# An attention layer and two feed-forward layers on one core: more steps with two banks, statistics in halves, weight tiles in other steps, a packed mask, and a third value part formed by VectorE

## The reference

```python
s_g = scale * q_g @ k_all.T;  out_g = softmax(s_g) @ v_all          # k_all = [k_g, k_l]
s_ll = where(|i - j| <= 32, scale * q_l @ k_l.T, -1e9)
out_l = softmax([scale * q_l @ k_g.T, s_ll]) @ [v_g, v_l]
x = concat([out_g, out_l], axis=2)   # heads side by side: (4, 544, 512)
x = x + relu(layernorm(x) * g @ w_ch1) @ w_ch2                      # 512 -> 2048 -> 512
h = relu(x @ w_in)                                                  # 512 -> 1024
out = (h * sigmoid(conv3_along_sequence(h, conv_w))) @ w_out
```

## Time and profile before

| | us |
|---|---|
| median of three runs | 797.08 (796.56 to 798.47) |
| the profiled execution, its own time | 794.28 |
| its span, first to last instruction | 792.5 |
| TensorE busy | 747.4 (94% of the span) |
| VectorE busy | 414.7 (52%) |
| ScalarE busy | 341.0 (43%) |
| GpSimd busy | 286.1 (36%) |
| mean granted TensorE clock | 0.98 of full speed |

### The profile page before, as it was taken

How to read it: one execution, slowest core, us unless ns; L and a number is a source line. 1 busy time by engine, 2 the same in 40 slices (tenths; PEclk the granted TensorE clock), 3 DMA queues, 4 the chain that set the end, 5 groups by cost and what they waited for, 6 DMA issues and landing times.

```text
span 792.5 us, 16702 instructions
## 1 busy us (share of the span) xinstructions
PE 747.4 (94%) x6496; PEld 690.6 (87%) x6496; DVE 414.7 (52%) x1008; ACT 341.0 (43%) x854; POOL 286.1 (36%) x241
## 2 busy tenths in 40 slices
PE   3886799989999999999999999999999999999997
PEld 2785789988998999899998999888888999999997
DVE  4798765685557654542112131212237676676764
ACT  5897576656565654143212222111114434343343
POOL 4888766353445340043212343020102222222322
PEclk9996799999999999999999999999999999999999
DMA  8766765355534600336261684650524222220200
GB/s 231 201 183 186 229 174 170 94 184 149 148 89 140 203 26 27 96 114 194 66 199 54 164 234 134 160 189 27 160 84 117 76 86 77 67 83 32 86 30 28
DMA packets 92702, 98.84 MB, mean 125 GB/s; under 512 B 10832, under 2 KB 68304, under 8 KB 92624
## 3 DMA queue, kind: packets, MB, share of 16 engines
q1 hardware_dynamic: 92624, 97.78, 41.5%
HBM read 68.14 MB, written 29.62 MB: 123 GB/s over the span
## 4 chain that ended last, share of the span: by engine, by line
PE 82%; DVE 7%; ACT 4%; issue 3%; POOL 2%; DMA 1%; SPq 0%; ACTq 0%; POOLq 0%; DVEq 0%
PE u_ps L506 34%; PE y_ps L506 23%; PE s_ps L506 15%; PE t_ps L548 5%; PE o_ps L506 4%; DVE bst L800 1%; DVE m_sb L731 1%; DVE p_lo L746 1%; DVE ln_n L815 1%; POOL k_lo L1095 1%; DVE v_res L722 1%; POOL q_st L1102 1%; ACT p_hi L969 1%; ACT e_sb L943 1%; DMA k_raw<-in_kqT 1%
## 5 line engine op out<-in xcount | busy, mean ns | idle before, releaser
L837 DVE SCALAR_TENSOR_TENSOR hb<-u_ps,hb 128x384 fp32r<-128x384 f32 (+1 forms) x48 | 28.9, 602 | 176.2 <-ACT hb L1013 176.2
L1131 POOL TENSOR_TENSOR hb<-gated,hb 128x272 fp32r<-128x272 f32 x64 | 54.9, 859 | 154.0 <-ACT hb L1041 154.0
L1013 ACT ACTIVATE hb<-u_ps 128x384 fp32r<-128x384 f32 (+1 forms) x48 | 25.3, 527 | 176.1 <-PE u_ps L506 176.1
L506 PE MATMUL u_ps<-xc,w_hi 128*128 128x274 f32 x512 | 99.8, 289 | 0.0
L854 DVE SCALAR_TENSOR_TENSOR conv_h<-relu_h,conv_sb,conv_h 128x272 f32<-128x272 f32 x128 | 88.8, 694 | 4.5
L1095 POOL TENSOR_TENSOR k_lo<-k_raw,k_hi 128x736 fp32r<-128x736 f32 x31 | 58.7, 1894 | 79.1 <-ACT k_hi L925 77.8
L506 PE MATMUL u_ps<-xn,w_hi 128*128 128x256 f32 x448 | 86.5, 291 | 0.1
L1116 POOL TENSOR_TENSOR w_lo<-w_raw,w_hi 128x1024 fp32r<-128x1024 f32 x24 | 57.8, 2409 | 79.1 <-ACT w_hi L1003 79.1
L506 PEld LDWEIGHTS u_ps<-xc,w_hi 128*128 128x128 f32 x512 | 80.8, 189 | 0.2
L1027 ACT ACTIVATE relu_h<-u_ps 128x274 f32<-128x274 f32 x64 | 25.6, 400 | 120.7 <-PE u_ps L506 120.7
L506 PE MATMUL u_ps<-xc,w_lo 128*128 128x274 f32 x256 | 73.9, 289 | 0.0
(11 more groups left out here) (135 smaller groups left out, 2148.7 us busy)
## 6 DMA issues: line engine op xcount, KB each, us to landing
w_raw<-in_wall SPq DMA_DIRECT2D x24, 512.0 KB, 4.0
k_raw<-in_kqT SPq DMA_DIRECT2D x64, 184.0 KB, 3.4
xc<-y_parts SPq DMA_DIRECT2D x8, 1092.0 KB, 5.9
q_raw<-in_kqT SPq DMA_DIRECT2D x64, 136.0 KB, 2.9
v_raw<-in_vx SPq DMA_DIRECT2D x32, 260.0 KB, 3.4
y_parts<-yT SPq DMA_DIRECT2D x16, 512.0 KB, 3.7
xn_parts<-xn SPq DMA_DIRECT2D x14, 512.0 KB, 4.1
xb<-xn_parts SPq DMA_DIRECT2D x14, 512.0 KB, 6.6
```

The source lines that it names most:

```text
L506: return nc.tensor.matmul(out, lhsT, rhs, start=start, stop=stop)
L837: v.scalar_tensor_tensor(out=lo, in0=u_ps[n % 2][:, 0:width], scalar=0.0, in1=hi.bitcast(f32), op0=ALU.max, op1=ALU.subtract).then_inc(hlo ...
L1131: g.tensor_tensor(hb[sc % HSLOTS][:, 1, 0:CN], gated[sc % 2][:, :], hb[sc % HSLOTS][:, 0, 0:CN].bitcast(f32), ALU.subtract).then_inc(clo_o ...
```

## The change

- **Banks.** The second transpose bank is used for all transposes of steps below 23 (before: below 19), the second output bank up to output number 10 (before: 8).
- **Statistics.** `ln_sums` is split: `half_sums` takes the sums of 256 of the 512 columns after the first four heads (steps 11, 27, 43, 59) and of the other 256 in steps 19, 35, 51, 67; `variances` combines both.
- **Weight tiles.** The first eight are treated in steps 9, 12, 15, 17, 24, 25, 26 and 28, through three staging buffers; the third is the memory of `y1_sb`.
- **Mask.** It comes from the host as bf16 in three tiles and is loaded straight into place by one transfer of 192 KB in place of two of 256 KB and two casts.
- **Value parts.** `v_last` moves from GpSimd to VectorE, in the same odd steps, ahead of `half_sums` and `scale_up`. GpSimd's `q_low` no longer waits for it.
- **Transfers.** The first four query transfers are issued by ScalarE. The last output is stored in four transfers, each as its part is copied.

```diff
-T_BANK = [k % 2 if T_STEP[k] < 19 else 0 for k in range(len(T_SEQ))]
+T_BANK = [k % 2 if T_STEP[k] < U0 else 0 for k in range(len(T_SEQ))]
...
-O_FLIP = 8
+O_FLIP = 10
...
-W_STEP = [13 + 2 * j for j in range(8)] + [70 + 2 * j for j in range(8)] + [U0 + N1 + 4 + 2 * j for j in range(8)]
+W_STEP = ([9, 12, 15, 17, 24, 25, 26, 28] + [70 + 2 * j for j in range(8)]
+          + [U0 + N1 + 4 + 2 * j for j in range(8)])
+W_SLOT = [j % 3 for j in range(8)] + [j % 2 for j in range(16)]
...
-        maskb = sb(ctx, "maskb", [P, 2, 512], bf16)
+        maskb = sb(ctx, "maskb", [P, 3, 256], bf16)
-        bst = sb(ctx, "bst", [P, QT, 6])
+        bst = sb(ctx, "bst", [P, QT, 2, 6])
...
             def w_load_step(j):
-                return 7 if j < 2 else W_STEP[j - 2] + 2
+                return 3 + 2 * j if j < 3 else W_STEP[W_BEFORE[j]] + 2
...
+                else:
+                    for m in range(KT):
+                        sp.wait_ge(oe_ok, KT * cc + m + 1)
+                        sp.dma_start(outT[b][:, m, CN * c:CN * (c + 1)], y_sb[:, m, :]).then_inc(out_out, 16)
...
-            load_q(0)
             load_k(0)
-            for u in range(2):
-                sp.dma_start(mask_raw[u], maskp[:, u, :]).then_inc(mask_in, 16)
+            sp.dma_start(maskb[:, :, :].bitcast(f32), maskp).then_inc(mask_in, 16)
             load_k(1)
-            load_q(1)
...
+            def v_last(m):
+                r = m % VSLOTS
+                dve.wait_ge(vres_ok, m + 1)
+                v.tensor_tensor(low(v_res[r]), v_res[r][:, :], top(v_res[r]), ALU.subtract).then_inc(vend_ok, 1)
...
+            def half_sums(b, half):
+                dve.wait_ge(o_ok, o_head(HEADS * b + GH * half + 3) + 1)
+                if half == 0 and b > 0:
+                    dve.wait_ge(lnn_ok, QT * b)
+                for t in range(QT):
+                    v.bn_stats(bst[:, t, half, :], x_loc[b % 2][:, t, 256 * half:256 * (half + 1)]).then_inc(stat_ok, 1)
...
+                if s % 2 == 1 and s // 2 < NHEADS:
+                    v_last(s // 2)
                 if s % 2 == 0 and 0 <= (s - 4) // 2 < NHEADS:
                     read_out((s - 4) // 2)
+                if s % 16 == 11 and s // 16 < BATCH:
+                    half_sums(s // 16, 0)
                 if s % 16 == 3 and 1 <= s // 16 <= BATCH:
-                    ln_sums(s // 16 - 1)
+                    half_sums(s // 16 - 1, 1)
+                    variances(s // 16 - 1)
...
+            for m in range(2):
+                act.dma_start(q_raw[m][0:D, :], kqT[m, :, KW:KQW]).then_inc(q_in[m], 16)
+                act.dma_start(q_raw[m][D:P, :], kqT[m, :, KW:KQW]).then_inc(q_in[m], 16)
...
-                if s % 2 == 1 and s // 2 < NHEADS:
-                    v_last(s // 2)
-                    if (s + 4) // 2 < NHEADS:
-                        pool.wait_ge(vend_ok, s // 2 + 1)
-                        q_low((s + 4) // 2)
+                if s % 2 == 1 and (s + 4) // 2 < NHEADS:
+                    pool.wait_ge(klo_ok, (s + 3) // 2)
+                    if min(W_STEP) < s:
+                        pool.wait_ge(wlo_ok, sum(step < s for step in W_STEP))
+                    if s % 16 == 3 and 1 <= s // 16 <= BATCH:
+                        pool.wait_ge(rstd_ok, s // 16)
+                    q_low((s + 4) // 2)
```

More of the change, by code:

```diff
@@ L143, in stats_before @@
 def stats_before(b):
-    return 9 * b
-W_STEP = [13 + 2 * j for j in range(8)] + [70 + 2 * j for j in range(8)] + [U0 + N1 + 4 + 2 * j for j in range(8)]
+    return 13 * b
+W_STEP = ([9, 12, 15, 17, 24, 25, 26, 28] + [70 + 2 * j for j in range(8)]
+          + [U0 + N1 + 4 + 2 * j for j in range(8)])
 W_AT = {s: j for j, s in enumerate(W_STEP)}
+W_SLOT = [j % 3 for j in range(8)] + [j % 2 for j in range(16)]
+W_USE = [W_SLOT[:j + 1].count(W_SLOT[j]) for j in range(24)]
+W_BEFORE = [max([i for i in range(j) if W_SLOT[i] == W_SLOT[j]], default=-1) for j in range(24)]
 def attention_mlp(nc, kqT, vx, wall, gln, convw, ident, maskp, outT):
@@ L194, in attention_mlp @@
         h_lo = [sb(xs, f"h_lo{r}", [P, 2 * P], f32r) for r in range(HSLOTS)]
-        y1_sb = [sb(xs, f"y1_sb{r}", [P, DM]) for r in range(2)]
+        y1_sb = sb(xs, "y1_sb", [P, 2, DM])
+        w_raw.append(y1_sb[:, :, :].rearrange("p a b -> p (a b)"))
         x_glo = sb(xs, "x_glo", [P, D])
@@ L249, in attention_mlp @@
         yb = [y_ps[:, 0, :], y_ps[:, 1, :], s_ps[:, 0, :], s_ps[:, 1, :]]
-        mask_raw = [v_res[VSLOTS - 2 + u][:, 0:512] for u in range(2)]
         def g_ps(G):
             return y_ps if G < 2 else s_ps
-        mask_in, const_in, const_ok, mask_ok = sem("mask_in"), sem("const_in"), sem("const_ok"), sem("mask_ok")
+        mask_in, const_in, const_ok = sem("mask_in"), sem("const_in"), sem("const_ok")
         warm_ok = sem("warm_ok")
@@ L260, in attention_mlp @@
         v_in = [sem(f"v_in{r}") for r in range(VSLOTS)]
-        w_in = [sem(f"w_in{r}") for r in range(2)]
+        w_in = [sem(f"w_in{r}") for r in range(3)]
         khi_ok, qhi_ok, qghi_ok = sem("khi_ok"), sem("qhi_ok"), sem("qghi_ok")
@@ L998, in weights_hi @@
                     act.wait_ge(dn_ok, DN[N1])
-                raw = w_raw[j % 2]
+                raw = w_raw[W_SLOT[j]]
                 if j < 2 * HALF:
@@ L1106, in q_low @@
                 g.tensor_tensor(to, q_raw[m % 2][D:P, SL:S], to.bitcast(f32), ALU.subtract).then_inc(qglo_ok, 1)
-            def v_last(m):
-                r = m % VSLOTS
-                pool.wait_ge(vres_ok, m + 1)
-                g.tensor_tensor(low(v_res[r]), v_res[r][:, :], top(v_res[r]), ALU.subtract).then_inc(vend_ok, 1)
             def weights_lo(j):
@@ L1115, in weights_lo @@
                 pool.wait_ge(whi_ok, j + 1)
-                g.tensor_tensor(w_lo[at][:, :], w_raw[j % 2][:, :], w_hi[at][:, :].bitcast(f32),
+                g.tensor_tensor(w_lo[at][:, :], w_raw[W_SLOT[j]][:, :], w_hi[at][:, :].bitcast(f32),
                                 ALU.subtract).then_inc(wlo_ok, 1)
@@ L1120, in inverse_deviation @@
                 n = 1 if b == BATCH else QT
-                pool.wait_ge(stat_ok, stats_before(b) + 2 * n + 1)
+                pool.wait_ge(stat_ok, stats_before(b) + (3 if b == BATCH else 13))
                 g.tensor_tensor(rstd[:, 0:n], veps[:, 0:n], minus_half[:, 0:n], ALU.pow).then_inc(rstd_ok, 1)
```

68 lines of the change are left out of this document (32 added, 36 removed).

## The result

The changed kernel takes 802.34 us (median of 4 runs, 801.4 to 803.67), the kernel before beside it on the same chip 796.82 us (796.51 to 798.47). The ratio is 1.0071, with a 95% interval of 1.0054 to 1.0088: slower, where 791.6 us was forecast. The profiled execution has a span of 799.5 us, 7.0 more than before.

What follows compares the result with a forecast made beforehand. TensorE, busy 94% of the span, was taken as the bound, with the time to `up(0)` to be won. Terms -1.4 + 1.0 - 5.0 - 1.0 + 1.9 - 1.0 = -5.5 from 794.28, plus 2.8, gave 791.6 us; range 786 to 799.

Steps and rivals of the forecast that it cites:

- Value part, steps 3 to 16: Steps 3 to 16: GpSimd relieved of `v_last`, VectorE's added work just fits; +1.0 us, from -2 to +5.
- "slower" rival: Steps 3 to 22: VectorE becomes the bound as `v_last` waits for GpSimd subtractions; +8, in all 799.6 us; chance 0.15.
- Opening: Before step 3: keys arrive earlier with fewer transfers ahead; -1.4 us, between 0.5 (bytes decide) and 2.5 (issue decides).
- Steps 17 to 22: Banks, halved statistics and moved weight tiles shorten the chain before `up(0)`; -5.0 us, from -2 to -8.
- Step 25: G0's transposes no longer wait 1.12 us for a low part behind a weight cast; -1.0 us.
- Step 30: `up(7)` waits for weight tile 7, only two steps after its `scale_up`; +1.9 us, bounds +0.5 and +3.
- Steps 35, 51, 67: Halved statistics -1.1, `v_last` ahead +0.6: -0.5 us each in steps 35 and 51, nothing in 67.
- End: Last output stored in four transfers: issues start earlier, last lands about the same; 0, within 0.5 us either way.
- The clock rival: Steps 17 to 22: fewer waits give TensorE its full 2.4 GHz; 3.5 us more gain, 788 us; chance 0.20.

Runs made afterwards that it cites:

- e1: Changed kernel with `v_last` back on GpSimd in the same steps, all else as changed: 796.39 us, 0.9985 of the kernel before.
- e5: Changed kernel with `v_last` back on GpSimd and the first eight weight tiles in steps 13, 15, ... 27 as before: 790.18 us, 0.9919 of the kernel before.
- e11: Changed kernel with `v_last` on GpSimd and weight tiles in steps 9, 11, 15, 17, 24 to 27: 789.21 us, 0.991 of the kernel before.
- e9: Kernel before with `v_last` replaced by a one-input `bn_stats` on VectorE, third value part left out: 800.01 us, 1.0037 of the kernel before.
- e10: Changed kernel with `v_last` replaced by a one-input `bn_stats` on VectorE, third value part left out: 797.55 us, 1.0017 of the kernel before.
- e6: Kernel before with the bank changes alone (transpose banks and output bank flips): 795.07 us, 0.9984 of the kernel before.
- e4: Changed kernel with the first eight weight tiles in their old steps 13, 15, ... 27, three staging buffers kept: 798.7 us, 1.002 of the kernel before.
- e3: Changed kernel with weight tile 7 treated in step 27 in place of 28: 798.79 us, 1.0022 of the kernel before.
- e2: Kernel before with `v_last` moved to VectorE alone: 805.96 us, 1.0109 of the kernel before.
- e7: Changed kernel with `v_last` on VectorE in the even steps, right behind `v_residue`: 834.7 us, 1.0481 of the kernel before.
- e12: Changed kernel with `v_last` on GpSimd and weight tiles in steps 13, 15, 17, 19, 24 to 27: 789.27 us, 0.9909 of the kernel before.
- e8: e5 with a 416-byte pad that puts later buffers at their addresses in the kernel before: 788.51 us, 0.9905 of the kernel before.

## Why the prediction was wrong

**The step that failed** is the term "*Value part, steps 3 to 16*", +1.0 with bounds of -2 and +5. It measured +10.0, outside its bounds and 9.0 of the 12.5 us between the forecast sum (-5.5) and the measured span (+7.0). Three things were off in it.

- *The wait of `v_last`.* I let it meet "the last 0.3 to 0.5 us" of a subtraction. The mean over ten was 0.54 us, but it is made of six that lose 0.3 or less, one that loses 0.6 and three that lose 1.3: each meeting costs what is left of the other's instruction. I had the row that shows this, 2.15 us for a `scale_up`, and spread it thin.
- *The waits of the others.* I charged the wait to `v_last` alone. In steps 3 to 16 its seven lose 3.8 us, but the three `scale_up` lose 3.7, two of them because they stand right behind a `v_last` and GpSimd's waiting operation goes in between. 6.3 us of added work, and 3.8, 3.5 more than before, and 0.3 of `v_residue` make 13.9; VectorE's busy time rose by 13.3.
- *The weight tiles.* I costed the one tile more as 1.05 us of ScalarE and one `scale_up`. e1 against e5 says 7.6 us in steps 3 to 16 without any `v_last` on VectorE. e11 splits it: 4.0 are tile 1's even step, 3.6 are left for the added tile and the earlier places.

My "slower" rival had the right mechanism with a mean wait of 0.9 us and 799.6 us; the mean was 0.54, so by its own arithmetic it would not have decided. It came true because the same wait fell on `scale_up` as well, and because the weight steps cost by themselves. e9 and e10 rule out the simpler reading, that VectorE just had too much work. So the side on which the time fell was among the rivals, at a chance of 0.15, and the size came from terms that neither the forecast nor the rival had.

**The other terms:**

- *Opening*, -1.4: the size is right; whether the bytes or the issue decide was not tested. The instruction `row_max(3)` starts at 18.46 us on average in the ten kernels with the new opening (17.85 to 19.43), at 19.88 in the four with the old one (19.09 to 20.80). One pair of traces alone (-1.2) would have told little.
- *Steps 17 to 22*, -5.0 within -2 to -8: -2.8 in the changed kernel, -2.6 in e5. The banks give 1.5 of the 3.5 that I had put on them, since other waits take their place (e6). e5, which adds the halves of the statistics (and mask, opening and split store), is 1.1 us shorter than e6 there, as worked out for the halves. `ln_rows` falls by 0.45 (forecast 0.4), but that is luck: GpSimd's query subtraction still falls on the second of its two instructions (1.50 us, 1.49 before) and not on the first. The first lasts 0.54 in place of 0.99, because GpSimd no longer has `v_last` beside it. Had the weight steps not been moved, nothing would be left of the gain beside `v_last` (e4: 32.6 us).
- *Step 25*, -1.0: the wait fell from 1.12 to 0.48, so -0.6. In e5, with the old weight steps, it is 1.12 again: the cause was right.
- *Step 30*, +1.9: a wait of 2.93 in the changed kernel, 2.04 in e1, gone in e3. Right place and mechanism, a little small; steps 23 to 30 in all cost 3.5.
- *Steps 35, 51, 67*, -0.5, -0.5, 0: -1.0, -1.0, -0.5. I had charged `v_last` ahead of the statistics with 0.6; e5, which has none there, gains the same 1.0, so it costs nothing.
- *End*, 0: -1.1. From the last row of the third layer to the end it was 11.4 us before and 10.2 after, and it is so in e5 (-1.2). The four small stores are issued within 1.8 us, 0.45 each where I had taken 0.6, and land sooner than I had worked out; e2, e6 and e9, with the one large store, have 11.4.
- *The third layer*, not in the forecast: +1.1 us between its first and last row, spread evenly. It appears in the changed kernel, e1, e3, e4, e7, e9, e10, e11 and e12, not in before, e2, e5, e6 and e8. e9 has the old instructions there, e5 the new ones, so the edits don't decide it; the addresses don't either (e8). What does stays open.

The clock rival fell: steps 17 and 18 have a granted clock of 0.65, steps 19 to 22 0.74, which is above the 0.58 of before but not near 1.0. In the first stretch it was 0.87 in the changed kernel, 0.90 in e1 and 1.00 in e5, e9 and e11. The kernel before had 0.92 and the shortest stretch of all, e11 had 1.00 and a stretch 4.2 us longer, so the clock doesn't set its length; how much it adds to the loss no run separates.

## What to carry to other kernels

Before an operation with two SBUF inputs is moved to VectorE or GpSimd, look at what the other engine runs at that moment, and charge the whole rest of that instruction, to it and to the next such operation behind it; keep two of them from standing in a row on VectorE. Of the operations with one SBUF input `bn_stats` stood there at its own length in all 64 cases of e9 and e10, while the `tensor_scalar` of `ln_rows` waited, so look at the operation too. Work that is put earlier to unload a critical stretch costs in the stretch that takes it: in e11 against e5 3.6 us were lost in the one and 3.6 won in the other. So test each part of a combined change by itself: here two parts of six turned a gain of 1% into a loss of 0.7%.

## What the runs showed of the hardware

- VectorE and GpSimd took turns in these traces. When both had an operation with two SBUF inputs ready, the one that had waited went next: in e2 GpSimd's between `v_last` and `scale_up`, in e7 at 150.77 to 153.7 us. A wait lasted to the end of the other's instruction: `v_last` of 2.76 us in e2, 0.75 of it its own, waits 2.0 of the 2.39 us that GpSimd's takes.
- After a wait of 2.04 us in e1 in which TensorE worked 2.09 of 4 us, its granted clock was 0.57 from 132 to 136 us, near the lower of its two levels (1.2 GHz), and a pair of matmuls lasted 0.63 us in place of 0.40; after one of 2.93 us in the changed kernel, with 1.35 of 4.20 us worked, it stayed at 1.00. Busy time by stretch, e1 first, then the changed kernel:

```profile
128.00:132.00 4.00, 2.09 (x14) 1.64 (x12) 1.89 (x6) 3.35 (x9) 2.31 (x2) 1.00 0.92 261
132.00:136.00 4.00, 3.87 (x33) 3.77 (x34) 0.69 (x2) 1.08 (x2) 2.62 (x4) 0.57 0.64 209
```

```profile
134.00:138.20 4.20, 1.35 (x10) 1.03 (x9) 2.45 (x7) 3.40 (x9) 2.31 (x1) 1.00 0.88 291
138.20:142.00 3.80, 3.72 (x39) 3.42 (x40) 1.50 (x5) 1.08 (x2) 2.40 (x4) 1.00 0.17 47
```

The shorter wait cost more: from `up(6)` to `up(8)` e1 falls back 3.8 us against the kernel before, the changed kernel 3.2. What decides it stays open.
- The opening varies between executions: e1, e5, e8, e11 and e12 have the same instructions up to step 8, and `row_max(3)` starts between 17.85 and 19.01 us, a spread as large as most single terms of this sum.
